# A fused attention, SoLU and expert kernel: routing of tiles in fours, one weight split moved to early iterations, and another order of work in the expert stage

## The reference

```
attn_out = attention(q, k, v)                 # q pooled by 2; 2304 tokens x 512 after the heads are joined
# SoLU layer (x is 2304 x 512, w_in 512 x 1024, w_out 1024 x 512)
h    = x @ w_in
sm   = softmax(h);  solu = h * sm
ln   = (solu - mean(solu)) / sqrt(var(solu) + 1e-6) * g_ln
x    = ln @ w_out
# mixture of 8 experts (w1: 8 x 512 x 1024, w2: 8 x 1024 x 512)
xn = x / (norm(x) + 1e-6);  en = expert_emb / (norm(expert_emb) + 1e-6)
logits     = xn @ en.T / tau
expert_idx = argmax(logits, axis=1)
gate_w     = softmax(logits)[own expert]
out[mask e] = gate_w * (relu(x[mask e] @ w1[e]) @ w2[e])
```

## Time and profile before

| engine | busy us | share of the span |
|---|---|---|
| PE | 1112.5 | 95% |
| PEld (weight loads) | 869.7 | 74% |
| DVE | 786.8 | 67% |
| ACT | 624.8 | 53% |
| POOL | 463.5 | 40% |

### The profile page before, as it was taken

One profiled execution on the slowest core, in us unless ns is written; L12 is line 12 of the kernel. 1 busy time (PEld: TensorE's weight loads), 2 busy tenths in 40 slices (PEclk: granted clock), 3 DMA queues, 4 the chain that ended last, 5 costly groups with the idle time before them and its releaser, 6 DMA issues. The chain is left out here.

```text
span 1168.8 us, 20754 instructions
## 1 busy us (share of the span) xinstructions
PE 1112.5 (95%) x6615; PEld 869.7 (74%) x6615; DVE 786.8 (67%) x1965; ACT 624.8 (53%) x1344; POOL 463.5 (40%) x470
## 2 busy tenths in 40 slices
PE   7899999999999999999899988997889999999996
PEld 6677777777777777776588776785678878888885
DVE  6687777778777777877547999999783541414110
ACT  5676666667666666764464334343564642525221
POOL 6766556666655666633422332213121111111111
PEclk9899999999999999999999999998899999999999
DMA  5211112221211222001420000004356661511100
GB/s 137 67 41 55 39 52 62 61 63 41 58 38 51 62 62 62 21 15 79 145 82 19 19 19 27 19 19 171 101 201 224 203 234 37 191 37 37 48 28 2
DMA packets 55843, 85.60 MB, mean 73 GB/s; under 512 B 10094, under 2 KB 28526, under 8 KB 55600
## 3 DMA queue, kind: packets, MB, share of 16 engines
q1 hardware_dynamic: 51728, 72.91, 19.4%
q0 software_dynamic: 4000, 11.28, 3.0%
HBM read 74.73 MB, written 11.27 MB: 74 GB/s over the span
## 5 line engine op out<-in xcount | busy, mean ns | idle before, releaser
L569 DVE TENSOR_REDUCE maxes<-s_ps 128x1 f32<-128x384 f32 x432 | 226.3, 548 | 34.2 <-PE s_ps L416 23.7
L329 POOL TENSOR_SCALAR probs<-probs,recips 128x1152 f32<-128x1152 f32 x128 | 157.1, 1227 | 162.2 <-DVE recips L586 162.2
L416 PE MATMUL s_ps<-kq 128*128 128x384 f32 x768 | 197.6, 367 | 10.6 <-ACT probs L733 8.6
L595 DVE COPY pt<-even_ps 128x384 f32<-128x384 f32 x279 | 155.5, 557 | 77.5 <-PE even_ps L455 77.4
L489 PE MATMUL pv_ps<-pt,values 128*64 128x320 f32 (+1 forms) x1152 | 171.5, 418 | 1.2 <-DVE pt L595 0.7
L702 ACT COPY pt<-odd_ps 128x384 f32<-128x384 f32 x144 | 68.9, 479 | 133.1 <-PE odd_ps L455 133.1
L1079 POOL DMA_INDIRECT out<-junk,target_rows x25 | 26.5, 1060 | 268.8 <-ACT junk L1781 268.5
L416 PEld LDWEIGHTS s_ps<-kq 128*128 128x128 f32 x768 | 123.7, 192 | 12.0 <-ACT probs L733 8.2
L455 PE MATMUL even_ps<-ident,probs 128*128 128x128 f32 x693 | 130.2, 286 | 1.5 <-DVE pt L595 1.4
L455 PEld LDWEIGHTS even_ps<-ident,probs 128*128 128x128 f32 x693 | 81.9, 142 | 60.7 <-issue 51.2
L489 PEld LDWEIGHTS pv_ps<-pt,values 128*64 128x64 f32 x1152 | 70.4, 136 | 72.4 <-issue 35.6
(11 more groups left out here) (289 smaller groups left out, 2422.4 us busy)
## 6 DMA issues: line engine op xcount, KB each, us to landing
w_raw_e<-in_moe_w SPq DMA_DIRECT2D x60, 512.0 KB, 5.3
k_raw<-in_k SPq DMA_DIRECT2D x32, 288.0 KB, 2.8
values<-in_v SPq DMA_DIRECT2D x16, 576.0 KB, 3.9
token_rows<-x_rows SPq DMA_DIRECT2D x18, 256.0 KB, 2.0
q_raw<-in_q SPq DMA_DIRECT2D x32, 128.0 KB, 2.9
q_raw<-in_q SPq DMA_DIRECT2D x16, 256.0 KB, 3.0
w_raw<-in_moe_w_in SPq DMA_DIRECT2D x4, 512.0 KB, 6.0
w_raw<-in_moe_w_out SPq DMA_DIRECT2D x4, 512.0 KB, 4.0
```

The source lines that it names most:

```text
L329: nc.gpsimd.tensor_scalar(part, part, recips[:, par, s:s + 1], 1.0, ALU.mult, ALU.mult).then_inc(norm_done, 1)
L416: last = nc.tensor.matmul(bank[:, 0:chunk], left, right, start=(i == 0), stop=(i == len(parts) - 1))
L569: nc.vector.tensor_reduce(maxes[:, e, c:c + 1], bank, AX.X, ALU.max).then_inc(max_done, 1)
L595: nc.vector.tensor_copy(pt[(par + s) % 2][:, i * 3 * P:(i + 1) * 3 * P], bank[:, 0:3 * P]).then_inc(t_out[i], 1)
```

## The change

1. `batch = 4`: `route(a, b)` handles four tiles at once, after every fourth tile's eighth dot. The dot multiplies by the constant 1.0 and the factor `emb_stat[:, 3, :]` is applied to the logits in `route`, by one more instruction for four tiles.
2. The split of expert 0's w1 goes from iterations 5 to 8 into the loop passes `at` = 2 and 3, two chunks in each, and its lo part from POOL to DVE. POOL's 12 `row_pick` go behind the last solu tile.
3. Between layer and experts the second `rank_tiles` moves behind `late_dot(0)` on PE, and each `low_first` moves one place later.
4. Experts: in each tile, the row parts (`low_x`; `relu` and `high_x`) go ahead of the w1 split. The w2 split of t = 0 goes ahead of `low_h(1)`. `weigh()` and its exponential go from t = 1 to the start of t = 2, the factor matmuls behind `down_e(1)`, and tile 0 is scaled later. Buffers are placed elsewhere for it.

```diff
@@ build_moe
+    batch = 4
@@ gpsimd
-                if 5 <= at < 5 + part:
-                    c = at - 5
-                    pool.wait_ge(first_w1_hi, c + 1)
-                    lo = slot_at(1, 1, c)
-                    nc.gpsimd.tensor_tensor(
-                        w_split[:, lo:lo + chunk], first_raw[:, c, :],
-                        w_split[:, slot_at(1, 0, c):slot_at(1, 0, c) + chunk].bitcast(F32),
-                        ALU.subtract).then_inc(w1_lo_done, 1)
-                if at == last - 1:
+                if at == last:
                     pool.wait_ge(spots_ready, 1)
@@ tensor
                 if at == last + 2:
                     turn_rows(0)
-                    pe.wait_ge(routed, late)
-                    pe.wait_ge(spots_ready, 1)
-                    rank_tiles(early, late)
             late_dot(0)
+            pe.wait_ge(routed, late)
+            pe.wait_ge(spots_ready, 1)
+            rank_tiles(early, late)
...
+                if t >= 1:
+                    down_e(t - 1, *gone)
                 if t == 2:
                     pe.wait_ge(factors_picked, 1)
...
-                if t >= 1:
-                    down_e(t - 1, *gone)
@@ vector
-            def route(m):
+            def route(a, b):
+                across = [P, b - a, experts]
+                dve.wait_ge(dots_done, experts * b)
+                then(nc.vector.tensor_tensor(lg[:, a:b, :], lg[:, a:b, :],
+                                             emb_stat[:, 3, :].unsqueeze(1).broadcast_to(across), ALU.mult))
+                then(nc.vector.tensor_reduce(row[:, a:b], lg[:, a:b, :], AX.X, ALU.max))
+                choose(a, b)
+                    for m in range(a, b):
+                        nc.vector.tensor_tensor(before[:, m + 1, :], before[:, m, :], hot[:, m, :],
+                                                ALU.add).then_inc(routed, 1)
+                        dve.wait_ge(routed, m + 1)
...
                     nc.vector.scalar_tensor_tensor(
-                        out=junk[:, e % 2, :], in0=x_rows[:, m % ring, :], scalar=emb_stat[:, 3, e:e + 1],
+                        out=junk[:, e % 2, :], in0=x_rows[:, m % ring, :], scalar=1.0,
                         in1=emb[:, e, :], op0=ALU.mult, op1=ALU.mult, accum_out=lg[:, m, e:e + 1]).then_inc(dots_done, 1)
-                    if e == experts - 1:
-                        route(m)
+                    if e == experts - 1 and m % batch == batch - 1:
+                        route(m - batch + 1, m + 1)
...
+                if at in (2, 3):
+                    for c in range((at - 2) * part // 2, (at - 1) * part // 2):
+                        dve.wait_ge(first_w1_hi, c + 1)
+                        nc.vector.tensor_tensor(w_split[:, lo:lo + chunk], first_raw[:, c, :],
+                                                w_split[:, hi:hi + chunk].bitcast(F32),
+                                                ALU.subtract).then_inc(w1_lo_done, 1)
...
             for t in range(1, slot_tiles):
-                split_next(t, 0, w1_hi_done, w1_lo_done)
+                if t == 2:
+                    weigh()
                 if t + 1 < slot_tiles:
                     low_x(t + 1)
+                split_next(t, 0, w1_hi_done, w1_lo_done)
                 if t == 1:
-                    weigh()
+                    split_next(0, part, w2_hi_done, w2_lo_done)
                 low_h(t)
@@ scalar
             for t in range(1, slot_tiles):
-                split_next(t, 0, w1_hi_done, up_e_done, halves * t)
+                if t == 2:
+                    act.wait_ge(shifted, 1)
+                    nc.scalar.activation(work[:], work[:], ACT.Exp).then_inc(exped, 1)
                 relu(t)
                 if t + 1 < slot_tiles:
                     high_x(t + 1)
+                split_next(t, 0, w1_hi_done, up_e_done, halves * t)
```

More of the change, by code:

```diff
@@ L873, in build_moe @@
         junk_sq = sb("junk_sq", [P, d_ff], BF16)
+        small = junk_sq[:].bitcast(F32)
+        squares, logs = small[:, 0:2 * tiles], small[:, 2 * tiles:4 * tiles]
+        inv, inv2 = small[:, 4 * tiles:6 * tiles], small[:, 6 * tiles:8 * tiles]
+        norms, gates, rest = [small[:, (8 + i) * tiles:(9 + i) * tiles] for i in range(3)]
         x_in = sb("x_in", [P, 3, d_model])
@@ new lines, in choose @@
+            def choose(a, b):
+                across = [P, b - a, experts]
+                then(nc.vector.tensor_tensor(work[:, a:b, :], lg[:, a:b, :],
+                                             row[:, a:b].unsqueeze(2).broadcast_to(across), ALU.is_equal))
+                then(nc.vector.tensor_tensor(work[:, a:b, :], work[:, a:b, :],
+                                             lowest[:].unsqueeze(1).broadcast_to(across), ALU.mult))
+                then(nc.vector.tensor_reduce(rank[:, a:b], work[:, a:b, :], AX.X, ALU.max))
+                then(nc.vector.tensor_tensor(hot[:, a:b, :], work[:, a:b, :],
+                                             rank[:, a:b].unsqueeze(2).broadcast_to(across), ALU.is_equal))
@@ L1489, in _ @@
                                     ALU.max).then_inc(source_first_ready, 1)
[L1492 to L1499 removed]
+            choose(late, tiles)
             with nc.allow_low_precision("counts up to the number of tiles are exact in bfloat16"):
@@ L1560, in _ @@
             nc.vector.tensor_copy(target_rows[:], ends[:]).then_inc(targets_ready, 1)
-            dve.wait_ge(rows_squared, tiles)
-            for i in range(ring):
-                dve.wait_ge(rows_stored[i], 16 * len(range(i, tiles, ring)))
-            low_first(2)
+            low_first(1)
             def low(base, c):
@@ L1622, in _ @@
             low_h(0)
+            dve.wait_ge(rows_squared, tiles)
+            for i in range(ring):
+                dve.wait_ge(rows_stored[i], 16 * len(range(i, tiles, ring)))
+            low_first(2)
             low_first(3)
@@ L1696, in _ @@
                     square(junk_sq[:], solu[:, (at - 1) % 2, :], sq_solu[:, at - 1:at], y_squared)
-                if 5 <= at < 5 + part:
-                    c = at - 5
-                    act.wait_ge(first_raw_in[c], 16)
-                    hi = slot_at(1, 0, c)
-                    nc.scalar.activation(w_split[:, hi:hi + chunk], first_raw[:, c, :], ACT.Copy).then_inc(first_w1_hi, 1)
                 if live(at - 1):
@@ L1716, in _ @@
                         square(junk_sq[:, 0:d_model], emb[:, e, :], sq_emb[:, e:e + 1], emb_squared)
+                if at in (2, 3):
+                    for c in range((at - 2) * part // 2, (at - 1) * part // 2):
+                        act.wait_ge(first_raw_in[c], 16)
+                        hi = slot_at(1, 0, c)
+                        nc.scalar.activation(w_split[:, hi:hi + chunk], first_raw[:, c, :],
+                                             ACT.Copy).then_inc(first_w1_hi, 1)
                 if at == 2:
@@ L1794, in _ @@
                     high_x(t + 1)
+                split_next(t, 0, w1_hi_done, up_e_done, halves * t)
                 if t == 1:
-                    act.wait_ge(shifted, 1)
-                    nc.scalar.activation(work[:], work[:], ACT.Exp).then_inc(exped, 1)
+                    split_next(0, part, w2_hi_done, down_e_done, 0)
+                if t >= 3:
+                    scale(t - 1)
+                high_h(t)
                 if t == 2:
```

87 lines of the change are left out of this document (26 added, 61 removed).

## The result

The changed kernel takes 1157.78 us (median of 4 runs, 1155.49 to 1158.29) where the kernel before takes 1170.39 on the same chip: ratio 0.9889, 95% interval 0.9869 to 0.9909, 12.6 us less. Run again later the ratio is 0.9882 (0.9867 to 0.9897). 18.7 us were forecast: the direction is right and the time is inside the range of 1145 to 1160, but above the 1148 to 1156 of the forecast taken alone. The profiled execution took 1155.49 us, its span is 1153.8: 15 us under that of before. It is the fastest of the four; the other three took 1157.73 to 1158.29.

What follows compares the result with a forecast made beforehand. DVE was taken to be the slower engine in layer iterations 4 to 12, PE mostly the bound in the experts. Layer and tail 16.8 plus experts 1.9 gave 18.7 us off 1170.57: 1152 us, range 1145 to 1160.

Steps and rivals of the forecast that it cites:

- PE sets the pace to the end of the layer: Layer: DVE's iterations fall below PE's 12.05 us or catch up in the next; layer and tail give 16.8 us.
- The moved split starves no one: Layer, iterations 2 and 3: maximum(4) starts about 628.0, 5.3 us late, but PE doesn't see it; 0 to 0.4 lost.
- The rival at 1159: Layer: PE does wait for the 5.3 us that maximum(4) is late, plus 1.7 of slow clock; chance 0.10.
- The tail: End of layer: last maximum 15.9 us earlier, y_lo(17, 0) 17.0 earlier, dots beside row_pick stretched to 0.79, PE waits about 2.9.
- Experts, tile 3: up_e(3) can start at 870.5 instead of 874.14 at half clock and ends 6.3 us earlier (3.6 and 2.7).
- Tile 8: Experts: x_lo no longer stands behind the weight split, so PE's wait of 1.59 us goes.
- Tiles 7 and 18: Experts: the w1 split, now behind relu and x_hi, makes PE wait 1.9 us at each, 3.8 lost.
- Experts, tile 4: PE waits 0.6 us for relu(3) and 1.6 more for x_lo(4); 2.2 given back, up_e(4) starts 4.1 earlier.
- The prediction's own sign of being wrong: Wrong if PE stops in iterations 4 to 7, dots stay at 0.747, or expert tiles show granted clock 0.50.
- All at granted clock 1.00: Experts: the stops of about 2 us ahead of up_e(4) and 1.9 ahead of up_e(7) and up_e(18) leave the clock full.
- row parts free (1146): Experts: the three added waits don't come, as ACT and DVE overlap branches with waits; 7.9 us gained there; chance 0.18.
- DVE as the bound (1156): Layer: DVE still sets the pace if the per-partition scalar costs nothing or a batch costs 3.0; layer gives 13; chance 0.15.

Runs made afterwards that it cites:

- the gather early: Changed kernel with gather(4) issued ahead of scatter(0) on POOL and each later gather one place earlier: 1150.60 us, ratio 0.9821 to the kernel before.
- the second profile: Profiled execution of the unedited changed kernel, run again beside the experiments: median 1157.81 us, ratio 0.9882; experts' stretch 321.5 us.
- the layer's part alone: Changed kernel with the loops over the expert tiles put back as in the kernel before: 1154.38 us, ratio 0.9855 to the kernel before.

## Why the prediction was right, and where it failed

- *PE sets the pace to the end of the layer*: right. 17.1 us for 16.8. By the record's terms about 26 us leave DVE's iterations 4 to 17, and only 17 came off the time, since the passes end at 12.07. So the terms can't be priced one by one: batching alone gives 11.2 of the 17.1 and its absence takes 9.6, the absence of the split's new place 2.9, that of the dots' constant 0.6. Their own sizes held: 0.06 us a dot (0.747 to 0.684), 2.1 us a batch.
- *The moved split starves no one*: right; `maximum(4)` 628.36 for 628.0, no stop. The rival at 1159 falls.
- *The tail*: the total held, a term was too big. I stretched each dot beside `row_pick` to 0.79 and had PE wait 2.9; the dots take 0.68 and 0.76 in turn, the wait is 0.60. It is `row_pick` that stretches, from 8.95 us to 13.10. ACT's copy of the rows then ends last (1.31 and 1.30).
- *Experts, tile 3*: right. `up_e(3)` starts 34.65 us behind `up_e(0)`, 38.11 before, at full clock. *Tile 8*: its wait went. *Tiles 7 and 18*: 1.80 and 1.81 for 1.9.
- *Experts, tile 4*: here the step failed: "Something else is late next: ACT's order in tile 2", 2.2 us for `relu(3)` and `x_lo(4)`. With the gather early that wait doesn't exist, and `up_e(4)` starts 6.3 us sooner relative to `up_e(0)` (53.44 to 47.11), the whole of what tile 3 won. In the changed kernel it starts 1.1 sooner (52.34) where I had 4.1. I had followed `scale(0)` to the third tile as two instructions on ACT and not asked who waits for them: POOL's `scatter(0)`, and behind it in the queue `gather(4)`. That is 5.2 us in place of 2.2, 3.0 too few. 1.9 - 3.0 = -1.1, against -1.2 in the first profile. The prediction's own sign of being wrong, a granted clock of 0.50 in the expert tiles, showed too (864.10 to 867.30).
- *All at granted clock 1.00* after the waits of 1.9: true of the first profile, but not of the second nor of most others with this code, 1.5 us. The experts lost 2.7 in the second profile, which the bound of -3 still held. These two, 3.0 and 1.5, are most of the 5 to 6 us by which the medians (12.6 and 13.8 us less) fall short of 18.7; the total stayed inside the range because the range was wide, not because the experts' term was right.
- *The rivals*: row parts free (1146) is refuted by the two waits; DVE as the bound (1156) gives a near number by a wrong road, since the layer's part alone is 1154.4.

## What to carry to other kernels

When an instruction moves later on one engine, list who waits for it, and then what is queued behind each waiter: an in-order queue turns a late store into a late load. A stall that is removed may have been hiding things; look for what lands late under it. Where a stop of TensorE is left, several profiles are needed to price it, as one may show the rarer clock. And price the edits of an engine that is the bound together, up to the floor that the next engine sets: behind it, another 8 us of work saved (the dots) is worth 0.6 us of the layer here.

## What the runs showed of the hardware

- The same wait of TensorE, 1.80 or 1.81 us at tile 7, was followed by the full clock in one execution of the same program and by 0.57 over four us in another. Five of seven profiled executions with two such waits had one of them followed by the lower clock, two had none. It is worth about 1.5 us each time. Behind a stop of 3.62 us the lower clock came each time, with 0.56 to 0.80 as the mean of seven us.
- POOL's `row_pick` (a tensor and a scalar in, 0.71 us alone) and DVE's dots lengthen each other. Beside dots most of its instructions take 1.23 to 1.33 us, and every second dot takes 0.76 in place of 0.68:

```profile
788.40 13.10 POOL L1090 TENSOR_SCALAR row_pick<-count,spot 128x128 bf16<-128x128 f32 x12
```

```profile
789.27 0.76 DVE L1346 SCALAR_TENSOR_TENSOR junk<-x_rows,emb 128x512 f32<-128x512 f32 x1
...
789.96 0.68 DVE L1346 SCALAR_TENSOR_TENSOR junk<-x_rows,emb 128x512 f32<-128x512 f32 x1
```

- POOL's subtraction of two tensors costs a dot more: 1.8 us in place of 0.68 beside `x_lo`, and 2.46 in place of 0.75 beside the w1 low part (with the factor from memory).
- A factor read per partition makes a dot 0.06 us longer than a constant does: 0.747 against 0.684 us, in the changed kernel with and without that one edit.
